# Attention with top-32 masking and two MLPs: the two lanes of a step selected one after the other, with their own threshold, shift and denominator

## The chip, the cores and the metric

The kernel runs on one core of a Trainium2 chip. The metric is device time in microseconds (us), the median of the runs. The core has a matrix engine (PE, with weight loads shown as PEld), a vector engine (DVE), a scalar engine (ACT), GpSimd (POOL) and SyncE (SP), which issues most of the DMAs here. Each engine works through its own list of instructions in order, and semaphores hold an instruction until what it needs is there.

## The reference, cut to what matters

Three stages follow each other. The kernel does not run them one after the other; it interleaves them.

```
# attention: q, k, v are (4, 8, 576, 64) float32
scores = scale * q @ k.T                                  # 576 x 576 for each of the 32 heads
kth    = the 32nd largest score of each row
scores = where(scores >= kth, scores, -1e9) - max(scores)
attn   = exp(scores) / (sum(exp(scores)) + 1e-9)
x      = attn @ v                                         # heads side by side: 2304 x 512

# MLP 1: w_in 512 x 2048, w_out 2048 x 512
h = x @ w_in;  x = (h * sigmoid(h)) @ w_out

# MLP 2: w1, w2 512 x 1024, w3 1024 x 1024, w_out 1024 x 512
out = ((x @ w1) * (x @ w2)) @ w3 @ w_out
```

## The kernel before, in words

The 2304 rows are cut into 9 units of 256 rows. For each unit the attention runs over 8 heads; a unit and a head together are one step, and there are 72 steps. A step has two lanes of 128 rows, and lane `t = 2*s + lane` is the index that the semaphores count in. After the 8 steps of a unit, its MLP work is done in small pieces: 16 H (first product), 16 Y (second product), 8 A and 8 B (the two products of MLP 2) and 8 O (the last product, with `w3 @ w_out` multiplied out beforehand in the W34 pieces). The values are split into a high and a low part (`_hi`, `_lo`), so that each product is three matmuls; ACT rounds the high part, POOL or DVE subtracts it for the low part.

One lane goes through this chain:

- QK on PE writes the scores to PSUM (L929), SC on ACT copies them to SBUF (L722).
- TOP on DVE selects the 32 largest values of each row in seven instructions: MAX8 gives the 8 largest (L828), MATCH_REPLACE8 takes these out (L830; the profile shows its load of the values as MATCH_VALUE_LOAD), and so on: four MAX8 and three MATCH_REPLACE8. Each reads what the one before it on the same lane wrote, and waits for the semaphore `topk_step`.
- BOUNDS on POOL (L608, L613) makes the threshold and the shift for both lanes of the step in two small instructions.
- MASK on ACT (L730, a Prelu) drives every score below the threshold far down, EXP on ACT (L738) takes the exponential and sums it into `den`.
- DEN and RDEN on DVE (L837, L843) add the epsilon to the sums and take the reciprocals, for both lanes in one instruction each. NORM on POOL (L620) scales.
- T on PE transposes (L944, L945). EV on ACT rounds the transposed values to `pT` (L750 to L756); LO makes the low part, for lane 0 on DVE (L848, L850), for lane 1 on POOL (L627).
- PV on PE multiplies with the values (L958 to L965), XC on ACT and XS on DVE collect the result (L763, L859, L861), XH and XL split it for the MLP (L769, L633).

In the MLP, TH on ACT (L776) and G on DVE (L871) form the gate, GR on ACT and GL on POOL (L796, L639) split it. For A and B these are AC on ACT (L782) and BM on DVE (L878).

The order of each engine's list is fixed ahead: every piece has a position, and the list is sorted by it. A piece of step `s` stands at `s + LAG[kind]`; the MLP pieces stand at positions that `mlp_positions` spreads evenly, 8 steps to a unit, from `M0` on. So a position says what comes first on one engine, not when it runs. `dve_order` gives the TOP instructions of a step the positions `s + TOP_SPAN * (2*step + lane) / 14`: the two lanes alternate, instruction by instruction. `sp_order` places the loads: Q and K for later steps, and the weights w3T and wo2 for W34 among them.

Of the kernel before, what the change touches and what calls it, by code (L numbers as in the profile page):

```python
# [12 lines left out]
P = 128  # L13
# [8 lines left out]
STEEP = 1.0e30  # L22
# [109 lines left out]
M0 = 9.887  # L132
# [25 lines left out]
def mlp_positions():  # L158
# [11 lines left out]
TOP_SPAN = 0.754  # L170

LAG = {
    "Q": -3.084, "K": -3.868, "KB": -2.41, "V": -0.098, "VB": -0.992, "KS": -1.402, "VS": 2.578,
    "WS": -0.244, "WS_PACE": 1.004, "WS_LATE": 0.078, "LOD": 1.81, "WS_KEPT": 0.105, "W12": 6.815,
# [8 lines left out]
}  # L183


def pe_order():
    out = [(p, s) for s, p in MLP_AT.items()]
    for s in range(STEPS):
        out += [(s + LAG["QK0"], ("QK", 2 * s)), (s + LAG["QK1"], ("QK", 2 * s + 1))]
        out += [(s + LAG["T0"], ("T", 2 * s)), (s + LAG["T1"], ("T", 2 * s + 1)), (s + LAG["PV"], ("PV", s))]  # L190
# [20 lines left out]
def split_steps(q, k, v):  # L211
    out = []
    for s in range(STEPS):
        out.append((s + LAG[q], ("QR", s)))
    for e, (s, _, _, _, fresh) in enumerate(ENTRIES):
        if fresh:
            out += [(s + LAG[k], ("KR", e)), (s + LAG[v], ("VR", e))]
    return out


def act_order():
# [4 lines left out]
    for s in range(STEPS):  # L226
        for lane in range(2):
            out += [(s + LAG[f"{kind}{lane}"], (kind, 2 * s + lane)) for kind in ("SC", "MASK", "EXP", "EV")]
        out.append((s + LAG["XC"], ("XC", s)))
        if s % 2:  # L230
            out.append((s + LAG["XH"], ("XH", s // 2)))
# [857 lines left out]
```

## Time and profile before

| | |
|---|---|
| median of 3 runs | 1138.74 us (1138.3 to 1140.32) |
| profiled execution, its own time | 1139.89 us |
| span of its trace | 1138.0 us |
| PE busy | 1056.2 us (93%) |
| DVE busy | 930.9 us (82%) |
| ACT busy | 773.0 us (68%) |
| POOL busy | 621.1 us (55%) |
| DMA | 310.42 MB, mean 273 GB/s |

The profile comes from one execution; its trace spans 1138.0 us, and 1.89 us more belong to its time. Busy time is the time in which at least one instruction of the engine was running. Matmuls overlap each other in the record, so that a busy PE is not PE at its peak. The times at which an instruction stands are microseconds from the start of the span.

### The profile page before, as it was taken

The page shows a single profiled execution, that of the slowest core. Times are in us where ns is not written, and L with a number is a line of the kernel's source. Part 1 is how long each engine was busy: PE and PEld are TensorE (multiplying, and loading weights), DVE is VectorE, ACT ScalarE, POOL GpSimd, SP SyncE. Part 2 cuts the span into 40 slices and gives each one's busy share as a digit, 9 for nine tenths or more (in the row PEclk, how much of TensorE's full clock was granted, in tenths as well). Part 3 has the DMA queues.
Part 4 walks back from the last instruction along what each step waited for, and adds up shares of the span by engine and source line. Part 5 has one row for each costly group of instructions (what it writes and reads, how often), then busy time and mean ns, then how long its engine had stood idle before and what let it go on. Part 6 is the DMA issues. An engine that isn't in the chain of part 4 may idle for free.

```text
span 1138.0 us, 24334 instructions
## 1 busy us (share of the span) xinstructions
PE 1056.2 (93%) x7872; PEld 986.5 (87%) x7872; DVE 930.9 (82%) x2066; ACT 773.0 (68%) x1921; POOL 621.1 (55%) x803
## 2 busy tenths in 40 slices
PE   1998577899999999999999999999999999999898
PEld 1554477799999999999999999999999999999897
DVE  5698886798889999999999998989999999991110
ACT  4577767677777787777767777877677767764221
POOL 3566767766665455566645555666545545543211
PEclk9999679999999999999999999999999999999999
DMA  8987769986998599779966996899579847963972
GB/s 270 316 281 250 260 221 311 310 275 200 330 374 288 163 342 346 260 233 359 359 236 212 335 345 212 265 365 362 193 249 335 297 154 279 331 216 128 312 244 93
DMA packets 129053, 310.42 MB, mean 273 GB/s; under 512 B 14240, under 2 KB 43936, under 8 KB 128928
## 3 DMA queue, kind: packets, MB, share of 16 engines
q1 hardware_dynamic: 110112, 275.30, 71.8%
q10 hardware_dynamic: 18816, 33.56, 8.4%
q8 instruction: 65, 1.06, 0.4%
q14 instruction: 60, 0.49, 0.1%
HBM read 263.19 MB, written 45.61 MB: 271 GB/s over the span
## 4 chain that ended last, share of the span: by engine, by line
PE 72%; DMA 9%; POOL 4%; DVE 4%; issue 4%; ACT 4%; ACTq 2%; SPq 1%; POOLq 0%; DVEq 0%
PE ps_h L1033 6%; PE ps_h L1035 6%; PE ps_h L1034 6%; DMA win<-win_split 6%; PE ps_s L929 5%; PE ps_x L965 5%; PE ps_h L995 5%; PE ps_h L996 5%; PE ps_h L997 5%; PE ps_y L1017 4%; PE ps_y L1019 4%; PE ps_y L1018 4%; PE ps_t L944 4%; PE ps_y L1046 3%; PE ps_y L1047 3%
## 5 line engine op out<-in xcount | busy, mean ns | idle before, releaser
L828 DVE MAX8 top<-rest 128x8 f32<-128x576 f32 x432 | 309.9, 747 | 0.0
L639 POOL TENSOR_TENSOR g_lo<-gate,g_hi 128x256 fp32r<-128x256 f32 x216 | 160.0, 741 | 240.7 <-ACT g_hi L796 240.2
L830 DVE MATCH_REPLACE8 rest<-top,rest 128x576 f32<-128x576 f32 x288 | 212.9, 743 | 0.5
L995 PE MATMUL ps_h<-x_hi,win 128*128 128x256 f32 x576 | 167.9, 291 | 9.1 <-DMA win<-win_split 8.9
L1033 PE MATMUL ps_h<-x_hi,w_hi 128*128 128x256 f32 x576 | 166.1, 288 | 5.1 <-DVE x_lo L884 4.4
L627 POOL TENSOR_TENSOR pT<-p_raw,pT 128x640 fp32r<-128x640 f32 x72 | 113.4, 1575 | 103.1 <-ACT pT L756 103.1
L1017 PE MATMUL ps_y<-g_hi,wout 128*128 128x256 f32 x576 | 165.7, 288 | 1.1 <-POOL g_lo L639 1.0
L996 PE MATMUL ps_h<-x_lo,win 128*128 128x256 f32 x576 | 163.0, 283 | 0.0
L997 PE MATMUL ps_h<-x_hi,win 128*128 128x256 f32 x576 | 162.9, 283 | 0.0
L1035 PE MATMUL ps_h<-x_hi,w_lo 128*128 128x256 f32 x576 | 162.7, 282 | 0.0
L1034 PE MATMUL ps_h<-x_lo,w_hi 128*128 128x256 f32 x576 | 162.7, 282 | 0.0
L1018 PE MATMUL ps_y<-g_lo,wout 128*128 128x256 f32 x576 | 162.1, 281 | 0.0
L1019 PE MATMUL ps_y<-g_hi,wout 128*128 128x256 f32 x576 | 162.0, 281 | 0.0
L620 POOL TENSOR_SCALAR probs<-probs,rden 128x576 f32<-128x576 f32 x144 | 107.3, 749 | 50.4 <-DVE rden L843 48.8
L995 PEld LDWEIGHTS ps_h<-x_hi,win 128*128 128x128 f32 x576 | 110.2, 191 | 12.8 <-DMA win<-win_split 11.9
L828 DVE MAX8 top<-scores 128x8 f32<-128x576 f32 x144 | 105.1, 753 | 15.5 <-ACT scores L722 14.0
L796 ACT CAST g_hi<-gate 128x256 fp32r<-128x256 f32 x216 | 87.1, 403 | 44.9 <-DVE gate L878 21.4
L1033 PEld LDWEIGHTS ps_h<-x_hi,w_hi 128*128 128x128 f32 x576 | 109.8, 191 | 8.2 <-issue 6.0
L730 ACT ACTIVATE probs<-scores,bounds 128x576 f32<-128x576 f32 x144 | 104.9, 772 | 12.4 <-POOL shift L613 12.4
L871 DVE SCALAR_TENSOR_TENSOR gate<-gate,ps_h 128x256 f32<-128x256 f32 x144 | 59.4, 413 | 64.9 <-ACT gate L776 62.7
L738 ACT ACTIVATE probs<-probs,shift 128x576 f32<-128x576 f32 x144 | 110.8, 774 | 0.0
L996 PEld LDWEIGHTS ps_h<-x_lo,win 128*128 128x128 f32 x576 | 110.2, 191 | 0.7
(78 smaller groups left out, 2840.2 us busy)
## 6 DMA issues: line engine op xcount, KB each, us to landing
win<-win_split SPq DMA_DIRECT2D x135, 512.0 KB, 6.4
wout<-wout_split SPq DMA_DIRECT2D x135, 512.0 KB, 4.9
wout<-w_dram SPq DMA_DIRECT2D x72, 512.0 KB, 3.9
v_split<-v_dram SPq DMA_DIRECT2D x64, 320.0 KB, 5.2
k_split<-k_dram SPq DMA_DIRECT2D x64, 288.0 KB, 5.8
v_dram<-v_split SPq DMA_DIRECT2D x32, 320.0 KB, 6.1
k_raw<-kT SPq DMA_DIRECT2D x64, 144.0 KB, 5.4
k_dram<-k_split SPq DMA_DIRECT2D x32, 288.0 KB, 6.9
```

The source lines that it names most:

```text
L639: nc.gpsimd.tensor_tensor(g_lo[:, n % NR, :], gate[:, n % NG, :], g_hi[:, n % NR, :].bitcast(F32), ALU.subtract).then_inc(g_split, 1)
L828: nc.vector.max(best[:, 8 * n:8 * n + 8], sc if step == 0 else left).then_inc(topk_step, 1)
L830: nc.vector.match_replace(left, best[:, 8 * n:8 * n + 8], sc if step == 1 else left, BELOW_ALL).then_inc(topk_step, 1)
L995: nc.tensor.matmul(ps_h[:, f % 2, 0:UN], hi, xh, start=(c == 0), stop=False)
L996: nc.tensor.matmul(ps_h[:, f % 2, 0:UN], hi, xl, start=False, stop=False)
L997: m = nc.tensor.matmul(ps_h[:, f % 2, 0:UN], lo, xh, start=False, stop=(c == KC - 1))
L1017: nc.tensor.matmul(y, hi, gh, start=(f == 0 and d % 2 == 0), stop=False, skip_group_check=True)
L1018: nc.tensor.matmul(y, hi, gl, start=False, stop=False, skip_group_check=True)
L1019: m = nc.tensor.matmul(y, lo, gh, start=False, stop=(f == FC1 - 1), skip_group_check=True)
L1033: nc.tensor.matmul(ps_h[:, n % 2, 0:UN], hi, x2_hi[:, c, :], start=(c == 0), stop=False)
L1034: nc.tensor.matmul(ps_h[:, n % 2, 0:UN], hi, x2_lo[:, c, :], start=False, stop=False)
L1035: m = nc.tensor.matmul(ps_h[:, n % 2, 0:UN], lo, x2_hi[:, c, :], start=False, stop=(c == KC - 1))
```

## The change

The selection of a step goes through lane 0's seven instructions first and then through lane 1's. `topk_step` counts seven for each lane. `top`, `shift`, `den` and `rden` get four places of one lane each instead of two places of both lanes. BOUNDS is gone: MASK takes the 32nd value out of `top` as its bias, with a scale of -1 and a slope of 1/STEEP on the negative side, and EXP scales by -SCALE*STEEP; STEEP is now a power of two. The shift is one small POOL instruction for each lane (SHIFT), and EXP waits for it. DEN and RDEN become one instruction of one column for each lane. All positions are new, M0 and TOP_SPAN with them, and the first 8 steps have a table of their own, START_LAG.

```diff
-STEEP = 1.0e30
+STEEP = 2.0 ** 90
-M0 = 9.887
+M0 = 9.746
-TOP_SPAN = 0.754
+TOP_SPAN = 0.786
 LAG = {
-    "Q": -3.084, "K": -3.868, "KB": -2.41, "V": -0.098, "VB": -0.992, "KS": -1.402, "VS": 2.578,
-    "WS": -0.244, "WS_PACE": 1.004, "WS_LATE": 0.078, "LOD": 1.81, "WS_KEPT": 0.105, "W12": 6.815,
-    "W12_PACE": 1.013, "W12_LOAD": -2.1, "W34": 0.649, "W34_PACE": 0.792, "W34_HI": 1.012, "W34_LO": 1.32,
-    "W34_KEPT": 1.639, "WIN": -0.148, "WOUT": -0.294, "OUT": 4.528, "QK0": -0.963, "QK1": -0.565,
-    "T0": 1.437, "T1": 1.851, "PV": 2.294, "SC0": -0.721, "SC1": -0.43, "MASK0": 0.813, "MASK1": 0.819,
-    "EXP0": 1.046, "EXP1": 1.065, "BOUNDS": 0.577, "EV0": 1.512, "EV1": 1.982, "XC": 2.339, "XH": 2.464,
-    "QR": -1.733, "KR": -1.752, "VR": 1.27, "QL": -1.162, "KL": -1.713, "VL": 1.739, "NORM0": 1.266,
-    "NORM1": 1.456, "LO0": 1.133, "LO1": 1.977, "XL": 2.681, "DEN": 1.402, "RDEN": 1.464, "XS": 2.572,
-    "TH": 0.138, "GR": 0.342, "AC": 0.241, "GRB": 0.335, "X2H": 0.097, "OC": 0.347, "GL": 0.313,
-    "GLB": 0.326, "G": 0.423, "BM": 0.403, "X2L": 0.268,
+    "Q": -3.181, "K": -3.393, "KB": -2.449, "V": -0.087, "VB": 0.073, "KS": -1.659, "VS": 2.667,
+    "WS": -0.418, "WS_PACE": 0.986, "WS_LATE": 0.091, "LOD": 2.001, "WS_KEPT": 0.126, "W12": 7.135,
+    "W12_PACE": 0.926, "W12_LOAD": -1.786, "W34": 0.566, "W34_PACE": 0.791, "W34_HI": 0.69, "W34_LO": 1.622,
+    "W34_KEPT": 1.277, "WIN": 0.077, "WOUT": -0.084, "OUT": 6.782, "QK0": -1.01, "QK1": -0.67, "T0": 1.338,
+    "T1": 1.736, "PV": 2.119, "SC0": -1.02, "SC1": -0.341, "MASK0": 0.133, "MASK1": 0.547, "EXP0": 0.609,
+    "EXP1": 1.053, "EV0": 1.498, "EV1": 1.815, "XC": 2.077, "XH": 2.349, "QR": -1.618, "KR": -2.13,
+    "VR": 0.912, "QL": -1.325, "KL": -1.742, "VL": 1.543, "NORM0": 1.003, "NORM1": 1.398, "LO0": -0.142,
+    "LO1": 1.729, "XL": 2.269, "XS": 2.591, "TH": 0.074, "GR": 0.277, "AC": 0.178, "GRB": 0.198,
+    "X2H": 0.099, "OC": 0.128, "GL": 0.246, "GLB": 0.185, "G": 0.607, "BM": 0.526, "X2L": 0.558,
+    "SHIFT0": 0.383, "SHIFT1": 0.45, "DEN0": 1.155, "DEN1": 1.594, "RDEN0": 1.417, "RDEN1": 1.744,
+    "TOP": -0.137,
 }
+START_LAG = {
+    "QK0": -0.994, "QK1": -0.605, "T0": 1.272, "T1": 1.67, "PV": 2.039, "SC0": -0.931, "SC1": -0.725,
+    "MASK0": -0.226, "MASK1": 0.115, "EXP0": 0.688, "EXP1": 0.728, "EV0": 1.137, "EV1": 1.707, "XC": 2.064,
+    "XH": 2.203, "QR": -1.574, "KR": -1.914, "VR": 0.753, "QL": -1.469, "KL": -1.651, "VL": 1.003,
+    "SHIFT0": -0.204, "SHIFT1": 0.35, "NORM0": 0.934, "NORM1": 1.215, "LO0": 2.336, "LO1": 1.817,
+    "XL": 2.19, "TOP": -0.203, "DEN0": 1.249, "DEN1": 1.871, "RDEN0": 1.291, "RDEN1": 1.88, "XS": 2.563,
+    "LOD": 1.995, "Q": -3.625, "K": -3.882, "KB": -5.47, "V": -0.835, "VB": 0.037, "KS": -0.749,
+    "VS": 3.538,
+}
+def lag(kind, s):
+    return s + (START_LAG if s < H else LAG)[kind]
...
 def dve_order():
...
-        for step in range(7):
-            for lane in range(2):
-                out.append((s + TOP_SPAN * (2 * step + lane) / 14, ("TOP", s, step, lane)))
-        out += [(s + LAG[kind], (kind, s)) for kind in ("DEN", "RDEN", "XS")]
+        for lane in range(2):
+            out += [(lag("TOP", s) + TOP_SPAN * (7 * lane + step) / 14, ("TOP", 2 * s + lane, step)) for step in range(7)]
+            out += [(lag(f"{kind}{lane}", s), (kind, 2 * s + lane)) for kind in ("DEN", "RDEN")]
+        out.append((lag("XS", s), ("XS", s)))
...
-                elif kind == "BOUNDS":
-                    s = op[1]
-                    pool.wait_ge(topk_step, 14 * s + 14)
-                    if s >= 2:
-                        pool.wait_ge(masked, 2 * s - 2)
-                    nc.gpsimd.tensor_scalar(bounds[:, s % 2], top[:, s % 2, :, 0:TOPK:TOPK - 1], -SCALE, None,
-                                            ALU.mult).then_inc(bounds_ready, 1)
-                    pool.wait_ge(bounds_ready, s + 1)
-                    if s >= 2:
-                        pool.wait_ge(probs_ready, 2 * s - 2)
-                    nc.gpsimd.tensor_tensor(shift[:, s % 2, :], bounds[:, s % 2, :, 0], bounds[:, s % 2, :, 1],
-                                            ALU.subtract).then_inc(bias_ready, 1)
+                elif kind == "SHIFT":
+                    t = op[1]
+                    pool.wait_ge(topk_step, 7 * t + 7)
+                    if t >= 4:
+                        pool.wait_ge(probs_ready, t - 3)
+                    nc.gpsimd.tensor_scalar(shift[:, t % 4, :], top[:, t % 4, TOPK - 1:TOPK], top[:, t % 4, 0:1], SCALE,
+                                            ALU.subtract, ALU.mult).then_inc(shift_ready, 1)
...
                 elif kind == "NORM":
-                    pool.wait_ge(rden_ready, s + 1)
+                    pool.wait_ge(rden_ready, t + 1)
...
                 elif kind == "MASK":
-                    act.wait_ge(bias_ready, s + 1)
+                    act.wait_ge(topk_step, 7 * t + 7)
...
-                                         bias=bounds[:, s % 2, lane, 1:2], scale=SCALE, alpha=STEEP).then_inc(masked, 1)
+                                         bias=top[:, t % 4, TOPK - 1:TOPK], scale=-1.0, alpha=1.0 / STEEP).then_inc(masked, 1)
                 elif kind == "EXP":
                     act.wait_ge(masked, t + 1)
-                    if s >= 2:
-                        act.wait_ge(den_ready, s - 1)
+                    act.wait_ge(shift_ready, t + 1)
+                    if t >= 4:
+                        act.wait_ge(den_ready, t - 3)
...
                 if kind == "TOP":
                     if step == 0:
                         dve.wait_ge(scores_copied, t + 1)
-                        if s >= 2:
-                            dve.wait_ge(bounds_ready, s - 1)
+                        if t >= 4:
+                            dve.wait_ge(masked, t - 3)
+                            dve.wait_ge(shift_ready, t - 3)
                     else:
-                        dve.wait_ge(topk_step, 14 * s + 2 * (step - 1) + lane + 1)
+                        dve.wait_ge(topk_step, 7 * t + step)
...
                 elif kind == "DEN":
-                    dve.wait_ge(probs_ready, 2 * s + 2)
-                    if s:
-                        dve.wait_ge(rden_ready, s)
-                    nc.vector.tensor_scalar(den_eps[:, :], den[:, s % 2, :], EPS, None, ALU.add).then_inc(den_ready, 1)
+                    dve.wait_ge(probs_ready, t + 1)
+                    nc.vector.tensor_scalar(den_eps[:, t % 2, :], den[:, t % 4, :], EPS, None, ALU.add).then_inc(den_ready, 1)
                 elif kind == "RDEN":
-                    dve.wait_ge(den_ready, s + 1)
-                    if s >= 2:
-                        dve.wait_ge(normed, 2 * s - 2)
-                    nc.vector.reciprocal(rden[:, s % 2, :], den_eps[:, :]).then_inc(rden_ready, 1)
+                    dve.wait_ge(den_ready, t + 1)
+                    if t >= 4:
+                        dve.wait_ge(normed, t - 3)
+                    nc.vector.reciprocal(rden[:, t % 4, :], den_eps[:, t % 2, :]).then_inc(rden_ready, 1)
```

The other orders take `lag(kind, s)` in the place of `s + LAG[kind]`, and otherwise stay as they are.

## Rows read from the trace of the kernel before

**Rows 1.** The page: busy totals, and the chain that ended last, by engine.
```profile
PE 1056.2 (93%) x7872; PEld 986.5 (87%) x7872; DVE 930.9 (82%) x2066; ACT 773.0 (68%) x1921; POOL 621.1 (55%) x803
...
PE 72%; DMA 9%; POOL 4%; DVE 4%; issue 4%; ACT 4%; ACTq 2%; SPq 1%; POOLq 0%; DVEq 0%
```
**Rows 2.** Busy time by stretch: PE, PEld, DVE, ACT, POOL, clock, DMA.
```profile
12.00:125.00 113.00, 86.97 (x315) 49.35 (x315) 94.16 (x202) 73.21 (x169) 68.77 (x79) 0.97 0.89 287
125.00:251.00 126.00, 98.83 (x690) 92.49 (x691) 99.50 (x221) 90.87 (x220) 89.69 (x102) 0.88 0.82 277
251.00:1009.00 758.00, 749.17 (x5968) 730.50 (x5967) 708.80 (x1579) 563.57 (x1423) 426.40 (x569) 1.00 0.84 285
1009.00:1138.00 129.00, 119.91 (x900) 113.20 (x899) 28.49 (x67) 42.18 (x107) 33.17 (x44) 1.00 0.55 188
```
**Rows 3.** DVE in order of time: starts, durations, idle time before.
```profile
601.11 0.75 DVE L828 MAX8 top<-scores 128x8 f32<-128x576 f32 x1
601.79 0.07 DVE L830 MATCH_VALUE_LOAD rest<-top,scores 128x8 f32 x1
...
609.39 0.29 DVE L859 TENSOR_TENSOR x_raw<-ps_x,x_raw 64x128 f32<-64x128 f32 x1 [0.79 <-ACT x_raw L763]
609.72 0.42 DVE L861 TENSOR_TENSOR x_raw<-ps_x,x_raw 64x256 f32<-64x256 f32 x1
...
1027.62 0.17 DVE L837 TENSOR_SCALAR den_eps<-den 128x2 f32<-128x2 f32 x1 [3.38 <-ACT probs L738]
1027.82 0.17 DVE L843 RECIPROCAL rden<-den_eps 128x2 f32<-128x2 f32 x1
```
**Rows 4.** DVE groups by line and shape: busy us, mean ns, idle before.
```profile
L828 DVE MAX8 top<-rest 128x8 f32<-128x576 f32 x432 | 309.9, 747 | 0.0
L837 DVE TENSOR_SCALAR den_eps<-den 128x2 f32<-128x2 f32 x72 | 25.2, 349 | 4.5 <-ACT probs L738 4.5
```
**Rows 5.** Line L837 alone: shortest, median and longest in ns.
```profile
L837 DVE TENSOR_SCALAR den_eps<-den x72: 154/164/864, 29.3 to 1027.6; 128x2 f32<-128x2 f32 x72
```
**Rows 6.** POOL and DVE together in order of time, from 299.3 us.
```profile
299.74 0.74 POOL L639 TENSOR_TENSOR g_lo<-gate,g_hi 128x256 fp32r<-128x256 f32 x1 [0.25 <-ACT g_hi L796]
299.77 0.74 DVE L837 TENSOR_SCALAR den_eps<-den 128x2 f32<-128x2 f32 x1
300.42 0.75 DVE L828 MAX8 top<-rest 128x8 f32<-128x576 f32 x1
```
**Rows 7.** Waits of all engines: who waited for whom, us, times, longest.
```profile
POOL bounds L608 <- DVE top L828: 71.4, 43, 4.6
ACT probs L730 <- POOL shift L613: 12.4, 23, 2.5
```
**Rows 8.** The first 43 us in order of time: SP, POOL, ACT, PE, DVE.
```profile
26.07 3.44 SPq L456 DMA_DIRECT2D q_raw<-qT  x1
...
16.63 0.73 POOL L571 TENSOR_TENSOR q_lo<-q_raw,q_hi 128x256 fp32r<-128x256 f32 x1
...
34.94 0.40 ACT L663 CAST q_hi<-q_raw 128x256 fp32r<-128x256 f32 x1 [6.34 <-DMA q_raw<-qT]
35.61 0.63 ACT L722 COPY scores<-ps_s 128x576 f32<-128x576 f32 x1
...
29.15 5.20 PE L977 MATMUL ps_y<-wo_sb,w3T_sb 128*128 128x512 f32 x8 [8.34 <-DMA w3T_sb<-w3T]
...
40.58 0.69 DVE L848 TENSOR_TENSOR pT<-ps_t,pT 128x512 fp32r<-128x512 f32 x1 [6.45 <-ACT pT L756]
42.22 1.41 DVE L828 MAX8 top<-scores 128x8 f32<-128x576 f32 x2
```
**Rows 9.** The second unit, 125 to 251 us: waits of DVE and of PE.
```profile
DVE gate L871 <- ACT gate L776: 17.4, 12, 4.1
...
PE ps_t L944 <- DVE pT L850: 11.8, 3, 4.2
```
**Rows 10.** ACT in order of time near 171 us.
```profile
171.60 0.41 ACT L796 CAST g_hi<-gate 128x256 fp32r<-128x256 f32 x1 [3.52 <-issue]
```

More of the change, by code:

```diff
@@ L227, in act_order @@
         for lane in range(2):
-            out += [(s + LAG[f"{kind}{lane}"], (kind, 2 * s + lane)) for kind in ("SC", "MASK", "EXP", "EV")]
-        out.append((s + LAG["XC"], ("XC", s)))
+            out += [(lag(f"{kind}{lane}", s), (kind, 2 * s + lane)) for kind in ("SC", "MASK", "EXP", "EV")]
+        out.append((lag("XC", s), ("XC", s)))
         if s % 2:
-            out.append((s + LAG["XH"], ("XH", s // 2)))
+            out.append((lag("XH", s), ("XH", s // 2)))
     for m in range(FC2):
@@ L251, in pool_order @@
         for lane in range(2):
-            out += [(s + LAG[f"{kind}{lane}"], (kind, 2 * s + lane)) for kind in ("NORM", "LO")]
-        out.append((s + LAG["BOUNDS"], ("BOUNDS", s)))
+            out += [(lag(f"{kind}{lane}", s), (kind, 2 * s + lane)) for kind in ("SHIFT", "NORM", "LO")]
         if s % 2:
-            out.append((s + LAG["XL"], ("XL", s // 2)))
+            out.append((lag("XL", s), ("XL", s // 2)))
     for (kind, u, f), p in MLP_AT.items():
@@ L290, in sp_order @@
             continue
-        out += [(s + LAG["K" if fresh else "KB"], ("K", e)), (s + LAG["V" if fresh else "VB"], ("V", e))]
+        out += [(lag("K" if fresh else "KB", s), ("K", e)), (lag("V" if fresh else "VB", s), ("V", e))]
     for e, (s, _, b, _, fresh) in enumerate(ENTRIES):
         if fresh:
-            out += [(s + LAG["KS"], ("KS", e)), (s + LAG["VS"], ("VS", e))]
+            out += [(lag("KS", s), ("KS", e)), (lag("VS", s), ("VS", e))]
     for n in range(2):
@@ L336, in build @@
         scores, probs = sb("scores", [P, 4, S]), sb("probs", [P, 4, S])
-        rest, top = sb("rest", [P, 2, S]), sb("top", [P, 2, 2, TOPK])
-        bounds, shift = sb("bounds", [P, 2, 2, 2]), sb("shift", [P, 2, 2])
-        den, den_eps, rden = sb("den", [P, 2, 2]), sb("den_eps", [P, 2]), sb("rden", [P, 2, 2])
+        rest, top = sb("rest", [P, 2, S]), sb("top", [P, 4, TOPK])
+        shift = sb("shift", [P, 4, 1])
+        den, den_eps, rden = sb("den", [P, 4, 1]), sb("den_eps", [P, 2, 1]), sb("rden", [P, 4, 1])
         p_raw, pT = sb("p_raw", [P, 2, KCH, P]), sb("pT", [P, 2 * KCH, UN], F32R)
@@ L618, in _ @@
                     s, lane = divmod(t, 2)
-                    pool.wait_ge(rden_ready, s + 1)
-                    nc.gpsimd.tensor_scalar(probs[:, t % 4, :], probs[:, t % 4, :], rden[:, s % 2, lane:lane + 1], 1.0,
+                    pool.wait_ge(rden_ready, t + 1)
+                    nc.gpsimd.tensor_scalar(probs[:, t % 4, :], probs[:, t % 4, :], rden[:, t % 4, :], 1.0,
                                             ALU.mult, ALU.mult).then_inc(normed, 1)
@@ L725, in _ @@
                     t = op[1]
-                    s, lane = divmod(t, 2)
-                    act.wait_ge(bias_ready, s + 1)
+                    act.wait_ge(topk_step, 7 * t + 7)
                     if t >= 4:
@@ L816, in _ @@
                 if kind == "TOP":
-                    s, step, lane = op[1:]
-                    t = 2 * s + lane
-                    sc, left, best = scores[:, t % 4, :], rest[:, lane, :], top[:, s % 2, lane, :]
+                    t, step = op[1:]
+                    sc, left, best = scores[:, t % 4, :], rest[:, t % 2, :], top[:, t % 4, :]
                     if step == 0:
                         dve.wait_ge(scores_copied, t + 1)
-                        if s >= 2:
-                            dve.wait_ge(bounds_ready, s - 1)
+                        if t >= 4:
+                            dve.wait_ge(masked, t - 3)
+                            dve.wait_ge(shift_ready, t - 3)
                     else:
-                        dve.wait_ge(topk_step, 14 * s + 2 * (step - 1) + lane + 1)
+                        dve.wait_ge(topk_step, 7 * t + step)
                     n = step // 2
```

26 lines of the change are left out of this document (13 added, 13 removed).

## The prediction

> **What bounds the kernel now.** I read the page first, then busy time by stretch, then DVE in order of time, then the waits. On the page PE is busy 93% of the span and holds 72% of the chain that ended last; DVE follows with 82% [rows 1]. The total hides that the span has four parts, and the reader is to see in [rows 2] how differently they stand.
>
> - 12 to 125 us is about the first 8 steps, without any MLP work. PE is idle 26.0 us of 113, DVE 18.8.
> - 125 to 251 us is about the second 8 steps, with the first MLP work beside the splitting of weights. PE is idle 27.2 us of 126, DVE 26.5, and the granted clock is 0.88: PE's gaps cost it twice.
> - 251 to 1009 us is the steady part, steps 16 to 71. PE is idle 8.8 us of 758, so PE is the bound. DVE is idle 49.2 us, 0.88 us of a step of some 13.6 us: it has just enough room.
> - 1009 to 1138 us is MLP alone, with DVE nearly empty. Nothing of the change reaches it except through the order of PE.
>
> PE's amount of work is the same after the change. So the time moves by what PE's idle time moves: it can shrink in the first two parts, and it grows in the third if DVE no longer has room.
>
> **The change on DVE: what the order costs.** In [rows 3] a MAX8 starts at 601.11 and the next DVE instruction at 601.79, before the 0.75 us are over: the two overlap by 0.07 (the unrounded times give 0.083 for nearly all such pairs). That is possible because the lanes alternate, and the next one needs only what was written one instruction earlier. Where an instruction needs the one right before it, there is no overlap but a gap: L859 ends at 609.68 and L861, which waits for it, starts at 609.72; DEN ends at 1027.79, RDEN starts at 1027.82, 0.03 later. A pair that becomes dependent costs 0.083 + 0.031 = 0.115 us. The trace has no dependent pair of MAX8 and MATCH_REPLACE8, so the ends are 0 (the semaphore is seen at once and the overlap stays) and 0.2 (twice the gap and more); I take 0.115, since the pairs L859/L861 and L837/L843 agree within 0.01.
>
> One lane after the other makes six such pairs in a lane, twelve in a step, unless another DVE instruction stands between them. Putting the positions of the diff in order gives, for step 31: three TOP of lane 0, LO of step 29, BM, three TOP, DEN, the seventh TOP; then lane 1: TOP, BM, two TOP, RDEN, three TOP, XS, TOP. Seven of the twelve pairs remain. Counted so, 506 remain in all: 75 in steps 0 to 7, 53 in steps 8 to 15, 378 in steps 16 to 71. In the old order there is none. That is 506 x 0.115 = 58 us of DVE time.
>
> Two more small instructions a step (one DEN, one RDEN) hold the engine some 0.07 us each, 10 us in all, since after a DEN at its short length the next instruction starts 0.07 us later. In 56 lanes RDEN now stands right behind its DEN: 6.4 us. The sum over the kernel is 75 us; on the steady part 43.5 + 7.8 + 5 = 56 us, on the first 8 steps 10.5, on the next 8 steps 8.
>
> **DEN's length.** Its mean is 349 ns, its median 164 [rows 4, 5]: 25.2 us less 72 x 0.164 is 13.4 us of something else. [Rows 6] shows what. A POOL instruction runs from 299.74 to 300.48, DEN starts at 299.77 and ends only at 300.51. Of the 72, 25 are over 0.5 us, 23 of them in the steady part (12.5 us), and each ends with a POOL instruction. With twice as many DEN the wait could double, 12.5 us more; if it is tied to the form (two columns), it could vanish, 12.5 us less. Those are the ends. The trace has no DVE instruction of one column. I take the lower end, as RDEN, with the same two columns, never exceeds its short length, so that the wait hangs on the form and not on size; I weigh it as 6 to 4.
>
> The Trainium skill speaks to both costs. "VectorE: DVE Perf Modes", section "The DRAIN you can't avoid", says that a semaphore between chained DVE instructions costs nothing extra; by that the 58 us would be 0. The trace here does not agree for these lengths: 0.083 of overlap against a gap of 0.03. "SBUF — State Buffer", section "Who interferes with whom", says that a DVE instruction in a 2-port mode and a GpSimd instruction block each other, and "Advanced Engine Details and Errata", section "VectorE Performance Modes", asks for an even number of columns, or an odd one above 1; by that DEN of one column waits no more. The first half agrees with the row at 299.77, no run here shows the second.
>
> **What the steady part makes of it.** DVE's need was 708.8 us of 758. With 56 more and 12.5 less it is 752, and 6 us of room are left if every step could use every other's; with the DEN waits doubled it is 777, 19 over. Steps can't share freely. Taking the time from each step's first MAX8 to the next one's, and the idle time and DEN waits in it, the steps whose addition is larger than their room miss 8.2 us together; if the DEN waits stay as long as they are, 27.1. PE is the bound beside it, so what DVE misses is added. Ends -6 and +39 (27 and the doubled wait), taken +8.
>
> **What leaves the other engines.** POOL loses BOUNDS and its inner wait and gains one SHIFT a step; MASK starts straight from DVE. ACT waited 12.4 us in all for the shift [rows 7], beside work of its own in a part where it is 26% idle; I take 0, ends -2 and +5, the latter if EXP, with EV, SC and TH queued behind it on ACT, now waits for SHIFT behind a POOL instruction. TOP's new waits for MASK and SHIFT are on a lane two steps back: 0, as is `rden`'s.
>
> **The first 8 steps.** Here START_LAG removes a stall that [rows 8] shows. Q of step 3 is issued at 26.07, behind w3T loads; ACT waits 6.34 us for it, until 34.94, and the scores of step 2 are copied only at 35.61. Then DVE does not take them: LO of step 0 stands before TOP of step 2 in its list (1.81 against 2.0), waits 6.45 us, and TOP starts at 42.22. In the new list Q of step 3 (-0.625) stands just ahead of the first w3T (-0.6), and LO (1.995) stands behind four TOP of step 2 (from 1.797). QK of step 2 stays behind three W34 parts instead of two, and W34 waits for w3T until 29.15, so the scores come no earlier than 35; but TOP can start at about 36, 6 us sooner. What is late next is LO itself, and T of lane 1 on PE behind it. Against that stand 10.5 us more of DVE need in 18.8 us of idle time, which fit except in the first step. Taken -6, ends -12 (all idle time beyond the need but the first 12 us' share) and +3.
>
> **The second 8 steps.** The hand-over from the first unit to the MLP is shorter in the lists: XL of step 7 stands at 9.19 instead of 9.68, XH at 9.20 instead of 9.46, H at 9.746 instead of 9.887. PE waits 11.8 us for LO here and DVE 17.4 us for TH [rows 9]; ACT is held itself, 3.52 us and similar at each saved weight chunk [rows 10], and this stays (WS_KEPT 0.126 for 0.105). M0 alone is 0.14 of 15.8 us, 2.2 us; with the earlier XL I take -5, ends -18 (DVE idle 26.5 less its 8 more) and +4. For the MLP alone at the end I take -1, since its first pieces have moved ahead by those 0.14 steps.
>
> **Sum.** -6 - 5 + 8 - 1 = -4 on the profiled execution's 1139.89 us (span 1138.0), 1135.9. That execution is 1.15 above the median of the runs shown: 1134.7, said as 1134.5.
>
> **The rivals.**
>
> A. DVE becomes the bound (slower). The mechanism is the 378 pairs and the 112 small instructions in the steady part together with DEN's wait on POOL, if this remains. It decides from the point where a step's addition, 1.0 us, is more than its room, 0.88 us of idle time on the mean and under 0.5 in the shortest steps. Price: +27 to +39 there, -12 elsewhere: 1138.7 + 15 to + 27, centre 1156. For it: the room is thin and PE has none. Against it: the DEN waits may go.
>
> B. The gain at the start is swallowed. LO of lane 0 behind four TOP delays T of lane 1 by up to 2.9 us in PE's list, W34 is late by w3T, and unit 1 keeps its length; -2 there, +4 to +8 in the steady part: 1139 to 1145, centre 1140.
>
> C. The second unit recovers. If steps 11 to 13 fall to DVE's need, 107 us for the eight instead of 126: -6 - 18 + 8 - 2: 1120. For it: PE and DVE both idle there. Against: ACT's holds remain.
>
> D. No cost for dependent pairs, as the rule on semaphores would have it: then DVE has 12 us more room after the change than before, the steady part gives +0, and the sum is -12: 1126.7. The dependent pairs of [rows 3] speak against it: the kernel has 24 pairs L859/L861, all with a gap of 0.03 to 0.04 us.
>
> **How the numbers follow.** Forecast 0.38, A 0.27, B 0.15, C 0.14, D 0.06. Within 0.2% (2.3 us, about what a measurement of this kernel can tell from no change) lie a tenth of the forecast and half of B. Faster: 0.33 + C 0.14 + D 0.06 = 0.53 less a little of C gone wrong, 0.51; same 0.13; slower: A 0.27 + half of B + 0.02, 0.36. The range from C's 1120 less 3 to A's centre less 2: 1117 to 1154; the forecast's own is 1127 to 1137.
>
> **What would show it.** DVE: MAX8 to MATCH_VALUE_LOAD of one lane 0.03 us apart, busy 931 - 13 + 58 = 975 us or so, less than 60 us idle up to 1009. DEN: 144 instructions with no length over 0.3 us; if they still reach 0.7, rival A gains. TOP of step 2 starts before 38 us. Steady part: first MAX8 of step 16 to that of step 71 within 10 us of before; if it grows by 20, DVE is the bound and the prediction is wrong. If the first two units together do not fall by 8 us or more, its gain side is wrong.

## The result and the profile after

The kernel after takes 1161.8 us in the median of 4 runs (1158.31 to 1165.54), the kernel before beside it 1139.53 (1138.3 to 1141.98). The ratio is 1.0193, with an interval of 1.0156 to 1.023: slower by 22 us. The forecast of 1134.5 had the wrong sign, and the range ended at 1154. The rival nearest to it is A (given as centre 1156; its own ends, 1138.7 + 15 and + 27, are 1153.7 and 1165.7, and their middle is 1160). The profiled execution, the longest of the four, took 1165.54 us, with a span of 1163.7; before it was 1139.89 and 1138.0. So the lengths below add up to 25.7 us, 3 or 4 more than the medians.

The page after, busy totals and the chain that ended last. Against [rows 1] DVE has 51.1 us more, and PE's share of the chain has fallen from 72% to 50%, DVE's has risen from 4% to 22%.

```profile
PE 1065.6 (92%) x7872; PEld 991.5 (85%) x7872; DVE 982.0 (84%) x2210; ACT 780.0 (67%) x1921; POOL 628.3 (54%) x803
...
PE 50%; DVE 22%; DMA 12%; issue 6%; ACT 3%; POOL 3%; ACTq 1%; SPq 1%; POOLq 0%; DVEq 0%
```

Busy time by stretch, cut just ahead of the first MAX8 of steps 0, 8, 16 and 71 (window, length, then PE, PEld, DVE, ACT, POOL, clock, DMA share, GB/s). The last stretch so holds step 71's selection as well as the MLP alone. First the kernel before, cut in the same way (the stretches of [rows 2] have round ends):

```profile
12.50:124.90 112.40, 86.97 (x315) 49.35 (x315) 94.06 (x202) 72.61 (x168) 68.27 (x79) 0.97 0.89 287
124.90:251.60 126.70, 99.43 (x695) 93.09 (x696) 100.19 (x222) 91.57 (x222) 89.69 (x102) 0.88 0.82 276
251.60:1009.30 757.70, 748.87 (x5966) 730.20 (x5965) 708.50 (x1579) 563.04 (x1423) 426.60 (x570) 1.00 0.84 286
1009.30:1138.00 128.70, 119.61 (x898) 112.90 (x896) 28.20 (x66) 42.11 (x107) 32.97 (x43) 1.00 0.55 188
```

The kernel after:

```profile
12.00:118.40 106.40, 84.03 (x307) 47.18 (x308) 101.02 (x212) 71.13 (x162) 65.77 (x74) 1.00 0.88 291
118.40:253.10 134.70, 100.15 (x691) 94.25 (x691) 106.77 (x239) 93.73 (x224) 93.44 (x105) 0.82 0.79 266
253.10:1032.40 779.30, 758.31 (x5959) 733.55 (x5957) 743.94 (x1690) 569.06 (x1425) 433.06 (x573) 1.00 0.81 278
1032.40:1163.70 131.30, 121.75 (x916) 115.58 (x916) 30.26 (x72) 43.18 (x109) 33.02 (x43) 1.00 0.55 186
```

The first unit is 6.0 us shorter, the second 8 longer, the steady part 21.6 longer, the end 2.6 longer. In the steady part DVE is still idle 35.4 us of 779, and PE's idle time has grown from 8.8 to 21.0. The rest stands inside groups that count as busy. Counted from start to start of neighbouring PE instructions, T waits 8.8 us (0 before), the products with a loaded `win` 18.4 (11.0), those into ps_y 8.8 (5.2). These three rises make 19.8 of the 21.6.

DVE in order of time in step 40's selection (start, duration). What stands in [rows 3] as an overlap is a gap here: MAX8 ends at 601.41 and the load of its values starts at 601.44. Where another instruction stands between two of one lane, as L885 does, the overlap is still there: 601.52 + 0.74 is past 602.18.

```profile
600.65 0.76 DVE L837 MAX8 top<-rest 128x8 f32<-128x576 f32 x1
601.44 0.09 DVE L839 MATCH_VALUE_LOAD rest<-top,rest 128x8 f32 x1
601.52 0.74 DVE L839 MATCH_REPLACE8 rest<-top,rest 128x576 f32<-128x576 f32 x1
602.18 0.41 DVE L885 TENSOR_TENSOR gate<-gate,ps_h 128x256 f32<-128x256 f32 x1
602.51 0.15 DVE L844 TENSOR_SCALAR den_eps<-den 128x1 f32<-128x1 f32 x1
602.57 0.75 DVE L837 MAX8 top<-rest 128x8 f32<-128x576 f32 x1
```

The group of MAX8 and the line of DEN alone, which answer to [rows 4] and [rows 5]. MAX8 has a mean of 759 ns for 747. No DEN is long. The three figures of DEN are the shortest, the median and the longest.

```profile
L837 DVE MAX8 top<-rest 128x8 f32<-128x576 f32 x432 | 327.7, 759 | 9.6
...
L844 DVE TENSOR_SCALAR den_eps<-den x144: 127/143/154, 30.4 to 1057.5; 128x1 f32<-128x1 f32 x144
```

The start, answering to [rows 8]: the scores of step 2 are copied at 33.06 and taken at 34.67, ahead of LO.

```profile
33.06 0.64 ACT L732 COPY scores<-ps_s 128x576 f32<-128x576 f32 x1 [2.30 <-PE ps_s L936]
...
34.67 0.74 DVE L837 MAX8 top<-scores 128x8 f32<-128x576 f32 x1
...
37.95 0.68 DVE L855 TENSOR_TENSOR pT<-ps_t,pT 128x512 fp32r<-128x512 f32 x1
```

The waits of the steady part, 251 to 1032 us (us, times, longest). The first row was 5.7 us in 6 times before, and T's wait for DVE was not among the rows.

```profile
PE ps_h L1002 <- DMA win<-win_split: 12.1, 12, 2.0
...
PE ps_t L951 <- DVE pT L857: 2.7, 9, 0.4
```

### The profile page after: what moved, and what is told of

Read it like the earlier page. It is cut to its first block, busy times and chain, and to the rows that moved or that the text cites. A ratio compares the mean times of both kernels' runs of the same rounds, so it can differ in the third digit from the quotient of the medians.

```text
span 1163.7 us, 24471 instructions
## 1 busy us (share of the span) xinstructions
PE 1065.6 (92%) x7872; PEld 991.5 (85%) x7872; DVE 982.0 (84%) x2210; ACT 780.0 (67%) x1921; POOL 628.3 (54%) x803
## 4 chain that ended last, share of the span: by engine, by line
PE 50%; DVE 22%; DMA 12%; issue 6%; ACT 3%; POOL 3%; ACTq 1%; SPq 1%; POOLq 0%; DVEq 0%
DVE rest L839 9%; DVE top L837 9%; DMA win<-win_split 8%; PE ps_h L1040 4%; PE ps_h L1042 4%; PE ps_h L1041 4%; PE ps_s L936 4%; PE ps_x L972 3%; PE ps_h L1002 3%; PE ps_y L1024 3%; PE ps_t L951 3%; PE ps_y L1026 3%; PE ps_y L1025 3%; PE ps_h L1003 3%; PE ps_h L1004 3%
## 5 line engine op out<-in xcount | busy, mean ns | idle before, releaser
L837 DVE MAX8 top<-rest 128x8 f32<-128x576 f32 x432 | 327.7, 759 | 9.6
L951 PE MATMUL ps_t<-ident,probs 128*128 128x128 f32 x576 | 91.4, 283 | 39.0 <-DVE pT L857 19.6
L739 ACT ACTIVATE probs<-scores,top 128x576 f32<-128x576 f32 x144 | 111.8, 777 | 17.2 <-DVE top L837 11.1
L732 ACT COPY scores<-ps_s 128x576 f32<-128x576 f32 x144 | 91.4, 635 | 40.9 <-PE ps_s L936 35.0
L837 DVE MAX8 top<-scores 128x8 f32<-128x576 f32 x144 | 107.8, 748 | 12.4 <-ACT scores L732 12.3
L951 PEld LDWEIGHTS ps_t<-ident,probs 128*128 128x128 f32 x576 | 68.5, 145 | 55.4 <-issue 42.5
```

The costliest lines, as they stand in the source:

```text
L837: nc.vector.max(best[:, 8 * n:8 * n + 8], sc if step == 0 else left).then_inc(topk_step, 1)
L951: nc.tensor.transpose(ps_t[:, c, :], probs[:, t % 4, P * c:P * c + P], ident[:, :])
```

## The experiments

Twelve kernels, each with an edit of the kernel before or of the kernel after. Three theories stood at the outset: P, the dependent pairs are the price; L, the new lists are; W, among the lists, the places of the weight work. The other letters are explained where they are used. A dependent pair is two neighbours on DVE of which the second reads what the first wrote. The lengths below are those of the four stretches, from each kernel's one profiled execution. The times are medians. A ratio is against the kernel before, measured again beside it, and can differ by some 0.2% from the quotient of the medians. Of the tables the diffs show the changed entries alone.

### The order of the selection alone, in the kernel before

```diff
-out.append((s + TOP_SPAN * (2 * step + lane) / 14, ("TOP", s, step, lane)))
+out.append((s + TOP_SPAN * (7 * lane + step) / 14, ("TOP", s, step, lane)))
-dve.wait_ge(topk_step, 14 * s + 2 * (step - 1) + lane + 1)
+dve.wait_ge(topk_step, 14 * s + 7 * lane + step)
```

> The kernel before with one edit: the fourteen TOP instructions of a step stand lane after lane; all other positions, BOUNDS and the two-column DEN stay. Theory P (dependent pairs fill DVE): without changed positions more pairs stay uncovered than the 506 of the changed kernel, each 0.117 us, so DVE needs about 60 us more; the steady part grows by 20 to 35 us, and the whole is 1.5 to 3% slower (1157 to 1173). Theory L (the new lists are what costs): within 0.5% of before, and the steady part within 5 us. DEN keeps two columns, so by both theories some 25 of the 72 stay near 0.7 us.

Measured: 1155.0 us, ratio 1.0126 (1.0085 to 1.0167). The three other lengths stay within 1.4 us of before; the steady part alone grows, by 15.9:

```profile
250.90:1024.50 773.60, 756.75 (x5967) 732.59 (x5966) 739.37 (x1579) 565.32 (x1422) 426.87 (x570) 1.00 0.82 280
```

With old lists, old MASK and old DEN, the order costs 15.5 us; both the time and the growth of the steady part (15.9 us) stayed below what was expected (1157 to 1173, 20 to 35). It has 541 dependent pairs. DVE is idle 34.2 us of 773.6, as in the kernel after. Of its 72 two-column DEN 11 are over 0.5 us, where some 25 were expected.

### The same instructions and positions without the dependence, in the kernel after

```diff
-                    else:
-                        dve.wait_ge(topk_step, 7 * t + step)
+                    elif t == 0 or step >= 2:
+                        dve.wait_ge(topk_step, 7 * t + step - (t > 0))
+                    if t and step % 2 == 1:
+                        best = top[:, (t - 1) % 4, :]
-nc.vector.max(best[:, 8 * n:8 * n + 8], sc if step == 0 else left)
+nc.vector.max(best[:, 8 * n:8 * n + 8], sc)
```

(MATCH_REPLACE8 reads `sc` too.)

> The changed kernel, same lists and same number of instructions, but no TOP instruction needs the one right before it (save in the first lane): MAX8 and MATCH_REPLACE8 always read the scores, MATCH_REPLACE8 takes its values from the lane before, and each waits for the instruction two back. What it leaves out: the selection is not that of the 32 largest. Theory P (the dependent pairs make the steady part long): same-lane pairs overlap by 0.083 again, DVE busy about 940, the steady part falls from 779 to 755 to 762 us, the whole to 1140 to 1148. Theory L (the new lists do it, as the alternating version of the changed kernel suggests, whose steady part was 774 us with no pair left): the gaps go, but the steady part stays at 770 or more and the whole at 1152 or more. Both act: 762 to 770.

Measured: 1144.33 us (12 runs, 1139.68 to 1153.97), ratio 1.0051 (1.0027 to 1.0076). DVE near the same time, also in step 40, with the overlap back:

```profile
599.63 0.74 DVE L841 MATCH_REPLACE8 rest<-top,scores 128x576 f32<-128x576 f32 x1
600.29 0.75 DVE L839 MAX8 top<-scores 128x8 f32<-128x576 f32 x1
600.96 0.07 DVE L841 MATCH_VALUE_LOAD rest<-top,scores 128x8 f32 x1
```

Its two later windows show the steady part 11.3 us shorter than after, and the second unit 3.4:

```profile
118.40:249.70 131.30, 98.86 (x686) 93.28 (x685) 100.74 (x239) 93.24 (x223) 93.44 (x104) 0.82 0.81 275
249.70:1017.70 768.00, 755.01 (x5963) 735.07 (x5962) 704.50 (x1690) 566.43 (x1425) 433.55 (x573) 1.00 0.81 281
```

DVE has 929.3 us of busy time, 6 dependent pairs are left, and T waits for nothing in the steady part. PE's wait for `win` stays, 10.4 us in 11 times, so it does not hang on the pairs. The steady part fell less than theory P expected (755 to 762) and lies where both causes were to act (762 to 770). This profiled execution took 1151.08 us, 6.8 above the kernel's median, so the windows say where the time left and the medians how much: 1161.8 - 1144.33 = 17.5, by the ratios to the kernel before, 1.0193 and 1.0051, some 16, and by each median against its own kernel before (22.3 and 3.4) 19.

The two runs nearly make a square. Old lists: 1139.5 with alternating lanes, 1155.0 with one lane after the other. New lists and the rest of the change, the order kept: 1144.3 without the dependence, 1161.8 with it. The order costs 14 to 16 in the one, by ratio or medians, the dependence 16 to 19 in the other; everything else costs 3 to 8.

### The lanes in alternation again, in the kernel after

```diff
-TOP_SPAN * (7 * lane + step) / 14
+TOP_SPAN * (2 * step + lane) / 14
-dve.wait_ge(topk_step, 7 * t + step)
+dve.wait_ge(topk_step[t % 2], 7 * (t // 2) + step)
-"MASK0": 0.133, "SHIFT0": 0.383, "SC1": -0.341
+"MASK0": 0.54, "SHIFT0": 0.44, "SC1": -0.56
-"MASK0": -0.226, "SHIFT0": -0.204   (START_LAG)
+"MASK0": 0.11, "SHIFT0": 0.34
```

> The changed kernel with the TOP instructions of the two lanes alternating again, a semaphore for each lane; MASK and SHIFT of lane 0 stand just ahead of those of lane 1, and SC of lane 1 stands 0.22 earlier, since the alternating order needs it. Everything else of the change stays. Theory P: the pairs go (0 in the place of 506), DVE busy falls by 42 us to about 940, the steady part returns to 750 to 762 us, and the whole is 1138 to 1146, with the second unit still 8 us long of it. Theory L: the lists stay, so the time stays within 0.5% of 1162.

Measured: 1179.13 us, ratio 1.0345 (1.0301 to 1.039), a miss. No dependent pair is left, yet DVE now waits for scores. The first row is of 12 to 120 us, the second of 260 to 1020:

```profile
DVE top L837 <- ACT scores L732: 36.2, 9, 11.5
...
DVE top L837 <- ACT scores L732: 25.1, 28, 2.2
```

The new lists place the second lane's scores half a selection later, and the alternating order wants both at once. So this was no clean test of the pairs.

### DEN as two one-column instructions, in the kernel before

```diff
-nc.vector.tensor_scalar(den_eps[:, :], den[:, s % 2, :], EPS, None, ALU.add).then_inc(den_ready, 1)
+nc.vector.tensor_scalar(den_eps[:, 0:1], den[:, s % 2, 0:1], EPS, None, ALU.add)
+nc.vector.tensor_scalar(den_eps[:, 1:2], den[:, s % 2, 1:2], EPS, None, ALU.add).then_inc(den_ready, 1)
```

> The kernel before, with DEN as two instructions of one column instead of one of two columns; nothing else. Theory F (the wait on POOL hangs on the two-column form): none of the 144 DEN is over 0.3 us, where 25 of 72 were near 0.7; the 13.4 us of waiting go, DVE idle grows by as much, and the time stays within 0.3% of before or gains up to 0.4%, since PE is the bound in the steady part. Rival (placement beside POOL decides, not the form): some of them still reach 0.5 us or more.

Measured: 1140.98 us, ratio 1.0003 (0.9982 to 1.0024). One of the two lines alone, and the steady part's window:

```profile
L837 DVE TENSOR_SCALAR den_eps<-den x72: 135/144/158, 28.8 to 1032.2; 128x1 f32<-128x1 f32 x72
```

```profile
248.90:1013.80 764.90, 752.61 (x5965) 733.16 (x5964) 699.91 (x1634) 563.02 (x1423) 426.98 (x570) 1.00 0.83 283
```

The form decides: no length near 0.7 us is left, at the old places. DVE's busy time in the steady part falls by 8.6 us, and the median doesn't move. The steady part of this one execution is even 7.2 us longer than before; the execution took 2.9 us more than its kernel's median. Lengths of stretches from single executions scatter by several us.

### Old places of the weight work, in the kernel after

```diff
-"WS": -0.418, "WS_PACE": 0.986, "WS_LATE": 0.091, "WS_KEPT": 0.126, "W12": 7.135, "W12_PACE": 0.926, "W12_LOAD": -1.786
+"WS": -0.244, "WS_PACE": 1.004, "WS_LATE": 0.078, "WS_KEPT": 0.105, "W12": 6.815, "W12_PACE": 1.013, "W12_LOAD": -2.1
```

> The changed kernel with the old positions of the weight splitting alone (WS, WS_LATE, WS_KEPT, W12, its pace and load, WS_PACE). Theory W: the second unit grew by 8 us (126.7 to 134.7) because the weight pieces in ACT's list stand so that ACT waits for w_raw and TH behind it; with the old positions the second unit is 125 to 129 us long and the whole 6 to 9 us faster than the changed kernel (1153 to 1156). Rival G: LO of lane 0 and the dependent pairs make the second unit long; then it stays at 133 or more, and the time within 3 us of 1162.

Measured: 1210.85 us, ratio 1.0611 (1.0577 to 1.0644). The first unit is 143.1 us for 106.4. PE's largest wait there, 12 to 155 us:

```profile
PE ps_x L972 <- issue: 37.3, 6, 9.8
```

A miss by 55 us. The lists are made to fit each other; seven of the table's 68 entries taken back tell nothing of what those seven cost.

### Old places of the MLP loads, in the kernel after

```diff
-"WIN": 0.077, "WOUT": -0.084
+"WIN": -0.148, "WOUT": -0.294
```

> The changed kernel with the weight loads of the MLP (WIN, WOUT) at their old positions, 0.21 to 0.23 of a step earlier in SP's list. Theory S (7 of the 22 us that the steady part grew are PE waiting for win, 18.4 us against 11.0, since its load stands later in SP's list): the wait for win falls to 9 to 13 us, the steady part by 5 to 8 us, the whole by 0.5%. Rival: the loads are held by the free place in the ring and not by the list, and the time stays within 2 us of the changed kernel.

Measured: 1158.9 us, ratio 1.017 (1.014 to 1.02). The stalls at a loaded `win` in the steady part fall from 18.4 to 12.4 us, the part's length by 2.6. That is half of what was expected at most, and it can't be put down to the loads: the intervals of 1.017 and of the kernel after, 1.0193 (1.0156 to 1.023), overlap, and a run below that leaves these loads where they are ("WS_KEPT" at 0.165) has as small a wait and a part 4 us shorter than after. Its row of 251 to 1026.4 us, against 12.1 in 12 times in the kernel after:

```profile
PE ps_h L1002 <- DMA win<-win_split: 7.6, 9, 1.3
```

### LO earlier by 0.14 of a step from step 8, in the kernel after

```diff
-"LOD": 2.001
+"LOD": 1.86
```

> The changed kernel with LO of lane 0 on DVE ahead of the first TOP of the step from step 8 on (LOD 1.86 for 2.001), where it stood behind three of them. Theory T (T of lane 1 waits on PE for this LO; 21.8 us in the second unit, 8.8 in the steady part): these waits fall by at least half, the second unit by 6 to 10 us, the steady part by 3 to 6, the whole by 0.8 to 1.3%. Rival: LO then makes DVE wait for EV of lane 0, the TOP behind it start later, and nothing is gained (within 0.3% or slower).

Measured: 1243.52 us, ratio 1.0917 (1.0891 to 1.0943). The expected sign was wrong, and the rival's mechanism true at a size nobody had put down. The waits of DVE, 257 to 1111 us:

```profile
DVE pT L855 <- ACT pT L765: 82.6, 56, 3.7
```

Once in each of the 56 steps DVE stands 1.5 us at LO for ACT's EV, with the selection queued behind it. The steady part is 853.3 us long, 74 more.

### The new start, piecewise in the kernel before and in the kernel after

```diff
+START = {"Q": -3.625, "K": -3.882, "KS": -0.749, "QL": -1.469, "QR": -1.574, "LOD": 2.198}   (before, steps 0 to 7)
```

> The kernel before, alternating lanes and all, with six positions of START_LAG in its first 8 steps: the loads of Q and K, the saving of K, the rounding and splitting of Q, and LO of lane 0 placed behind the first TOP of the next but one step (2.198, which in this kernel's order is what 1.995 is in the changed one). Theory Q (the stall at 28 to 42 us is Q of step 3 issued behind w3T, and LO ahead of TOP): TOP of step 2 starts at 34 to 38 us in the place of 42.2, the first unit takes 105 to 109 us in the place of 112.4, the whole 0.3 to 0.6% less (1134 to 1138). Rival (the lane order made the first unit shorter, since lane 0 is ready 4.6 us sooner): the first unit stays at 111 or more.

Measured: 1164.09 us, ratio 1.0201 (1.0169 to 1.0234). The first unit is 128.4 us for 112.4; two of its waits, 12 to 125 us:

```profile
PE ps_t L951 <- DVE pT L857: 15.8, 5, 4.6
DVE w L872 <- ACT w L723: 14.9, 5, 8.5
```

A miss again. W34's pieces still stood where the old start wanted them, and DVE stood at one of them for 8.5 us.

```diff
-"LOD": 1.995, "Q": -3.625      (START_LAG, after)
+"LOD": 1.995, "Q": -3.084
```

> The changed kernel with the load of Q in the first 8 steps back at its old position (-3.084 for -3.625), so that Q of step 3 is issued behind three pieces of w3T again. Theory Q (this load made ACT wait until 34.94 us, and its early place is the larger half of the 5.8 us by which the first unit got shorter): ACT waits 4 us or more for q_raw before step 3, TOP of step 2 starts at 37 us or later in the place of 34.7, the first unit takes 109 to 113 us in the place of 106.6, the whole 0.2 to 0.5% more than the changed kernel. Rival O (only the place of LO ahead of TOP mattered): the first unit stays within 1.5 us.

Measured: 1159.69 us, ratio 1.0185 (1.0147 to 1.0223). Q of step 3 is issued as said, TOP of step 2 moves by 0.3 us only, and the first unit is 106.7 us long where theory Q wanted 109 to 113:

```profile
23.02 1.62 SPq L470 DMA_DIRECT2D q_raw<-qT  x1
...
34.97 0.74 DVE L837 MAX8 top<-scores 128x8 f32<-128x576 f32 x1
```

```diff
-"LOD": 1.995, "Q": -3.625      (START_LAG, after)
+"LOD": 1.79, "Q": -3.625
```

> The changed kernel with LO of lane 0 ahead of the first TOP of the next but one step in the first 8 steps (1.79 for 1.995), where it stood behind four of them. Theory O: DVE waits for EV of lane 0 before each of these steps, 3 us for the first (EV ends at 36.6 us, TOP could start at 34.7) and, from the same move at 8 to 71, where each step became 1.3 us longer, 1 to 2 us in each step: first unit 112 to 120 us, whole 0.5 to 1.1% more than the changed kernel. Rival: in the first unit, where DVE is idle for 5 us only and PE for 22, T of lane 1 is released earlier and makes up for it: within 2 us of 106.6.

Measured: 1177.56 us, ratio 1.0323 (1.0271 to 1.0376). The first unit is 126.7 us for 106.4. The wait at LO, 12 to 125 us, was 1.6 us in 3 times in the kernel after:

```profile
DVE pT L855 <- ACT pT L765: 17.1, 6, 4.9
```

Of the two edits that [rows 8] suggested, LO's place behind TOP is what the first unit of the new lists needs; Q's place is not. Both put into the old lists shortened nothing, so LO's place is not enough by itself.

### The saved weight chunks later, in both kernels

```diff
-"WS_KEPT": 0.126      (after)
+"WS_KEPT": 0.165
```

> The changed kernel with the saving of the late weight chunks (WSK on ACT) at 0.165 behind its Y piece in the place of 0.126, so that it stands behind the next TH and not just ahead of it. Theory K (the second unit is long since ACT stands in WSK, 3 to 4 us at each late chunk, for the POOL split of wout, and TH, G on DVE, LO behind G and T on PE wait in a row): the second unit falls from 134.7 to 126 to 130, ACT's waits before TH there from 11.2 to under 4 us, the whole by 0.4 to 0.7%. Rival: WSK then holds what stands behind it instead, and loads of w_raw come later; within 0.2% of the changed kernel.

Measured: 1159.92 us, ratio 1.0159 (1.0131 to 1.0186). The waits that this was to remove, in the kernel after, 125 to 251 us:

```profile
PE ps_t L951 <- DVE pT L857: 16.0, 4, 7.2
...
DVE gate L878 <- ACT gate L785: 15.8, 7, 6.0
...
ACT gate L785 <- issue: 11.2, 5, 4.1
```

The last row is gone. In its place, 118 to 250 us:

```profile
DVE pT L855 <- ACT pT L765: 11.7, 6, 4.3
```

The second unit is 132.2 us for 134.7, short of the 126 to 130 that were expected, and the whole is within the noise of the kernel after.

```diff
-"WS_KEPT": 0.105      (before)
+"WS_KEPT": 0.21
```

> The kernel before with the same move (0.21 for 0.105, which puts WSK behind the next TH here). Theory K: the waits of G for TH in its second unit (17.4 us) fall by at least half, the second unit from 126.7 to 119 to 123, the whole by 0.3 to 0.6% (1134 to 1137). Rival as in the changed kernel: within 0.2% of before.

Measured: 1144.97 us (12 runs), ratio 1.0026 (1.0002 to 1.005). It gives nothing there.

## Why the prediction was wrong

**The steady part: the term +8, the step that failed.** It measured +21.6. Two inputs were right. There are 506 dependent pairs, as counted, with a gap of 0.034 us and the overlap of 0.083 gone: 0.117 at the join for 0.115. DEN's waits vanished, as taken 6 to 4. What failed is the step behind them, DVE's need set against its room: "it is 752, and 6 us of room are left", and from it "the steps whose addition is larger than their room miss 8.2 us together".

The need itself was too small. Count as need the busy time and, with it, the gaps under 0.1 us between instructions that follow each other at once. It was 708.5 + 6.8 = 715.2 us before and is 743.9 + 20.9 = 764.9 after (unrounded): 13 more than 752, and 7 more than the 757.7 us that the whole stretch took before. Half of the 13 are the 6.8 us of gaps, which the prediction's 708.8 left out. The other half is that the need rose by 49.7 us for 43.5. Among it, a pair costs more than its join: a MAX8 that reads what its neighbour has just written takes 761 ns for 747, and from the load of the values to MATCH_REPLACE8 it is 78 ns for some 65. By busy time and gaps, the kernel after against the run without the dependence, a pair costs 0.14 us. DVE's total, forecast as 975, is 982.0; the forecast had counted the pairs' gaps as busy and left the added small instructions out.

The room was too large. DVE's longer waits, 42.4 us before, are still 14.4 after. In seven of the eight runs with the pairs they stay between 10.6 and 15.0 (the eighth, with LO at 1.86, has more), so they were not there to be filled. The order alone in the kernel before shows it by itself: a need of 759.8 us, only 2 above the old length, 13.8 us of waits, and a part 15.9 longer. T's waits on PE agree: 8.8 us for 0, and none without the dependence. That the pairs' time arrives late at ACT, POOL and PE ahead of DEN, the gates or LO, and comes back to DVE as these waits, is my reading; no run isolates it.

In the kernel before the order added 65 us of DVE time in all (541 pairs), in the kernel after the dependence 70 (500 pairs), and about a quarter of it shows. DVE is at 98% of the steady part after: by my own sign, a growth of 20, it is the bound. The end of 27.1 that I tied to DEN's waits was nearer than 8, though they went.

The size +21.6 comes from two executions. In four kernels with old lists and alternating lanes the steady part is 757.7 to 764.9 us long, in six with the new lists and the pairs 775.0 to 779.9 (LO at 1.86 apart): the growth is 10 to 22.

**The second unit: -5 forecast, +8.0 measured.** The sign is wrong. I argued from M0 and XL in the lists that the hand-over is shorter. XL of step 7 did come earlier, 148.4 for 150.2 us, and the first H on PE 152.5 for 153.5. Then it is lost: the first product of MLP 2 comes at 239.4 for 235.6. PE waits there for LO and DVE for TH, as in [rows 9], with 16.0 and 15.8 us for 11.8 and 17.4. ACT is still held at the saved chunks as in [rows 10], with 11.2 us, but by this kind of wait in all less than before (14.1 for 18.4). New is its wait for a load of `w_in`, 1.6 us in one time before (125 to 251 us):

```profile
ACT win L690 <- DMA w_raw<-w_in: 7.6, 3, 3.2
```

With PE's longer pauses goes a lower granted clock of this stretch, 0.82 for 0.88. The order is not the cause by itself: put alone into the kernel before, it leaves the unit at 125.8 for 126.7 us. Removing the dependence from the kernel after makes it 3.4 us shorter, the old load places 4.4, a later save 2.5, Q behind w3T 2.7, each in one profiled execution. Q's edit concerns the first 8 steps alone, and the profiled execution of the kernel after was 3.7 us above its median. So some 3 of the 8 us may belong to that execution, and none of the four edits can be credited. The remainder, some 5 us, lies with the new lists; which part of them stays open.

**The first unit: -6 forecast, -6.0 measured**, and the reason held: TOP of step 2 starts at 34.67 for 42.22 us, forecast at about 36. The agreement of the size is partly luck: with LO ahead of TOP again the unit is not 6 but 20 us longer, and in the old lists the new start made it 16 us longer. Also, the stretch ends at a MAX8, so part of its gain is selection running ahead of the rest. The start and both units together end at 253.1 us for 251.6. I had said that the gain side is wrong if the two units do not fall by 8; they grew by 2.0. Rival B named this outcome and had 0.15.

**The MLP alone: -1 forecast, +2.6 measured.** 1.9 of it lie in step 71's selection, which the stretch begins with. The rest was not studied.

**DEN and MASK.** One column is not held by POOL. That freed 12.5 us of DVE time, which I counted in full against the pairs; alone it is worth 0.3 us, 1.0003 with 0.9982 to 1.0024. So taking the 12.5 off the need was right as a sum of DVE time, and wrong as time gained: removed where DVE has room, they are worth nothing that can be measured. ACT's wait for the shift before MASK, 12.4 us in 23 times, became a wait for the selection, 11.1 us in 6 times; no run tells what that is worth.

**The lists and the rest, 3 to 8 us.** Where they lie is open. Three attempts to take parts of the lists back or over made things slower by 17 to 49 us than the kernel they were put into, so the parts can't be priced one by one.

**The weighing.** Rival A named the mechanism, DVE becoming the bound, at 0.27, and leaned on the DEN waits remaining. They went, and the cost came all the same, inside A's own ends of 1153.7 to 1165.7. Its centre should have read 1160, and the range, taken from it less 2, would then have ended at 1158, still short of 1161.8. (B's 1139 to 1145 has its middle at 1142, not 1140.) D is refuted by the order alone. The Trainium skill's rule in "VectorE: DVE Perf Modes", section "The DRAIN you can't avoid", that a semaphore between chained instructions costs nothing extra, would have made the order free; here a wait for the neighbour costs 0.117 us at each join and 15.5 us of the kernel's time, so the measurement decides against it for chains of this length. A semaphore by itself is as free as it says: in the run without the dependence most selection instructions still wait for one, set by the instruction before their neighbour, and the overlap of 0.083 is there. The Trainium skill says in "SBUF — State Buffer", section "Who interferes with whom", that a DVE instruction with at most one SBUF input, outside the 2-port modes, does not contend with GpSimd, and the Trainium skill's conditions for such a mode in "Advanced Engine Details and Errata", section "VectorE Performance Modes", leave out a single column. By that DEN would never be long, and all 144 are at most 154 ns.

## What to carry to other kernels

Two independent chains of selection instructions on DVE are worth interleaving: each instruction then starts before its neighbour ends, and what reads like "the same instructions in another order" cost 1.3% here. When an engine's need is compared with a stretch, count its short gaps too: they were 20.9 us here. And do not count its waits as room before you have asked which inputs they are for: 11 to 15 us of them could not be filled. An order list is tuned as a whole. Test it by changing what an instruction needs at the same place, as the run without the dependence did, and not by moving one place back.

## What the runs showed that was not expected

- One instruction moved ahead by 0.14 of a step costs 82 us of 1162, since it then stands 1.5 us ahead of its input in each of 56 steps; in the kernel before nearly the same place (1.81) does not.
- A MAX8 is itself longer when it reads what its neighbour has just written: 761 ns on the mean for 747, with the same size. Over all 432 that read `rest` the mean is 759, 5 us in sum. One that reads `scores` and feeds the next takes 749.
- In the steady part, with DVE at 93%, 8.6 us less on it moved nothing in the median, and 45 to 50 us more (busy time and short gaps) came with 16 to 22: the cost of added work near the bound isn't the mirror of the gain from removed work.
